# First stage of a long convolution: plain float32 fold, product on GpSimd, blocks made one ahead

## What is computed

```python
h_filt = (np.maximum(pos_emb @ w1, 0.0) @ w2) * window      # filter, 12480 x 128
u = x * v                                                   # 2 x 12480 x 128
y = irfft(rfft(u, 2 * S, axis=1) * rfft(h_filt, 2 * S, axis=0), axis=1)[:, :S]
x = (x * y).reshape(B * S, D)
h = x @ w_in
P = a[0] + a[1] * h + a[2] * h**2 + a[3] * h**3
Q = 1.0 + abs(b[0]) * abs(h) + abs(b[1]) * h**2
out = (P / (Q + 1e-6)) @ w_out
```

## Time and profile before

| | us |
|---|---|
| median of 3 runs | 2366.12 |
| lowest and highest run | 2360.96, 2369.22 |
| span of the profiled execution | 2364.7 |

### The profile page before, as it was taken

The page is one execution under the profiler, slowest core; times in us unless marked ns, Lnnn a source line. Parts: engine busy times, 40 slices in busy tenths (PEclk is TensorE's granted clock), DMA queues, the critical chain, the costliest instruction groups (busy, mean ns, idle before and its releaser), DMA issues.

```text
span 2364.7 us, 33272 instructions
## 1 busy us (share of the span) xinstructions
PE 2081.2 (88%) x8964; PEld 1464.9 (62%) x8964; DVE 2042.7 (86%) x2499; ACT 1993.8 (84%) x2670; POOL 1892.7 (80%) x1218
## 2 busy tenths in 40 slices
PE   7888578889877999999999999999999999999997
PEld 5666478889874555555555555555555555555554
DVE  3777566767666999999999999999999999999998
ACT  3677455555546999999999999999999999999998
POOL 3666367777755888888888888888888888888887
PEclk9999889999997999999999999999999999999999
DMA  6888655656552111111111111111111111111100
GB/s 163 246 257 263 206 128 146 154 139 162 137 127 60 29 29 28 28 31 28 31 48 28 28 28 28 28 28 28 31 28 32 48 28 28 28 28 28 28 11 11
DMA packets 65724, 175.02 MB, mean 74 GB/s; under 512 B 5046, under 2 KB 8414, under 8 KB 62686
## 3 DMA queue, kind: packets, MB, share of 16 engines
q1 hardware_dynamic: 65694, 174.67, 28.0%
HBM read 102.89 MB, written 71.76 MB: 74 GB/s over the span
## 4 chain that ended last, share of the span: by engine, by line
DVE 22%; ACT 20%; issue 11%; POOL 9%; PE 7%; ACTq 0%; DVEq 0%; DMA 0%; POOLq 0%
DVE g_s L735 9%; DVE lin L723 8%; ACT lin L634 6%; POOL den L609 6%; ACT mag L640 5%; ACT r_p L652 5%; DVE num L727 4%; PE m_p L790 3%; PE h_p L811 3%; POOL slope L601 3%; ACT den L645 3%; DVE xy_lo L714 1%; ACT xy_hi L625 0%; DVE oT L743 0%; ACT o_s L681 0%
## 5 line engine op out<-in xcount | busy, mean ns | idle before, releaser
L609 POOL TENSOR_TENSOR den<-slope,mag 128x832 f32<-128x832 f32 x480 | 944.6, 1968 | 43.4 <-POOL slope L601 6.9
L822 PE MATMUL acc_p<-g_s,w_out_s 128*128 128x416 f32 x1920 | 759.6, 518 | 18.3 <-DVE g_s L735 15.0
L601 POOL TENSOR_SCALAR slope<-mag,den_c 128x832 f32<-128x832 f32 x480 | 500.0, 1042 | 168.0 <-ACT mag L640 154.5
L723 DVE SCALAR_TENSOR_TENSOR lin<-lin,coef,h_p 128x832 f32<-128x832 f32 x480 | 516.4, 1076 | 33.9 <-ACT mag L640 33.9
L727 DVE SCALAR_TENSOR_TENSOR num<-lin,coef,h_p 128x832 f32<-128x832 f32 x480 | 518.8, 1081 | 17.0
L811 PE MATMUL h_p<-xy_hi,w_lo 128*128 128x416 f32 x960 | 406.5, 423 | 132.4 <-DVE num L727 110.2
L735 DVE SCALAR_TENSOR_TENSOR g_s<-num,coef,r_p 128x832 f32<-128x832 f32 x480 | 515.3, 1074 | 3.5 <-issue 1.8
L822 PEld LDWEIGHTS acc_p<-g_s,w_out_s 128*128 128x128 f32 x1920 | 346.9, 189 | 233.5 <-issue 210.8
L634 ACT ACTIVATE lin<-h_p,coef 128x832 f32<-128x832 f32 x480 | 458.0, 954 | 5.2 <-PE h_p L811 5.2
L645 ACT ACTIVATE den<-den 128x832 f32<-128x832 f32 x480 | 434.8, 906 | 27.4 <-POOL den L609 26.1
L811 PEld LDWEIGHTS h_p<-xy_hi,w_lo 128*128 128x128 f32 x960 | 180.7, 188 | 399.8 <-DVE num L727 384.2
(11 more groups left out here) (66 smaller groups left out, 2878.1 us busy)
## 6 DMA issues: line engine op xcount, KB each, us to landing
bent<-bent_s SPq DMA_DIRECT2D x60, 576.0 KB, 4.7
bin_s<-bent SPq DMA_DIRECT2D x24, 1440.0 KB, 12.6
x_s<-in_x SPq DMA_DIRECT2D x60, 416.0 KB
back<-back_s SPq DMA_DIRECT2D x24, 960.0 KB, 6.5
vin_s<-back SPq DMA_DIRECT2D x30, 768.0 KB, 5.8
v_s<-in_v SPq DMA_DIRECT2D x30, 416.0 KB
out<-o_s SPq DMA_DIRECT2D x60, 208.0 KB
pos_s<-in_pos_emb SPq DMA_DIRECT2D x30, 88.0 KB
```

What stands on the lines that cost most here:

```text
L601: nc.gpsimd.tensor_scalar(slope[:, q % DEEP], mag[:, q % DEEP], den_c[:, 1:2], den_c[:, 0:1], ALU.mult, ALU.add).then_inc(slope_done, 1)
L609: nc.gpsimd.tensor_tensor(den[:, q % DEEP], slope[:, q % DEEP], mag[:, q % DEEP], ALU.mult).then_inc(den_done, 1)
L723: nc.vector.scalar_tensor_tensor(out=lin[:, q % 2], in0=lin[:, q % 2], scalar=coef[:, 2:3], in1=h, op0=ALU.add, op1=ALU.mult).then_inc(qua ...
L822: mm = nc.tensor.matmul(acc_p[:, 0:TOK], w_out_s[:, ft], g_s[:, q % DEEP, t], start=(ft == 0), stop=(ft == FT - 1))
```

## The change

The fold takes plain float32 operands, one matmul for each half in place of three. The high and low copies of `fold` and `uh` and their four instructions per block are gone, with the two semaphores between them. The product runs on GpSimd. The preparation runs one block ahead (LEAD_MAKE 1) and the loads four (LEAD_LOAD 4). Fold 0 waits for the product and the filter of its block; product and filter wait for the folds of the block whose slot they overwrite. The thresholds of `split_done` in the later stages are two lower.

```diff
-            LEAD_LOAD, LEAD_MAKE, LEAD_SPLIT = 5, 2, 1
+            LEAD_LOAD, LEAD_MAKE = 4, 1
@@ gpsimd
-                def split_lo(i, s):
-                    for half in range(2):
-
-                        pool.wait_ge(uh_hi_done, (i * SLOTS + s) * 2 + half + 1)
-                        at = slice(half * (JB // 2), (half + 1) * (JB // 2))
-                        nc.gpsimd.tensor_tensor(uh_lo[:, s, at], uh[:, s, at], uh_hi[:, s, at].bitcast(F32),
-                                                ALU.subtract).then_inc(uh_lo_done, 1)
-
-                pipelined(pool, ITERS, SLOTS, [(0, split_lo)])
+                def product(i, s):
+                    blk = i * SLOTS + s
+                    pool.wait_ge(xv_in[s], 32 * (i + 1))
+                    if positive(blk - 1):
+                        pool.wait_ge(g_done, (blk - 1) * JB)
+                    nc.gpsimd.tensor_tensor(uh[:, s, :, 0:BD].rearrange("p j (b d) -> p b j d", b=BATCH),
+                                            x_s[:, s], v_s[:, s], ALU.mult).then_inc(prod_done, 1)
+
+                pool.wait_ge(pad_zero, SLOTS)
+                pipelined(pool, ITERS, SLOTS, [(LEAD_MAKE, product)])
@@ scalar
-                pipelined(act, ITERS, SLOTS, [(LEAD_MAKE, posT_copy), (0, cos_part(0)), (LEAD_SPLIT, split_hi(0)),
-                                              (LEAD_MAKE, relu), (0, cos_part(1)), (LEAD_SPLIT, split_hi(1)),
+                pipelined(act, ITERS, SLOTS, [(LEAD_MAKE, posT_copy), (0, cos_part(0)), (LEAD_MAKE, relu), (0, cos_part(1)),
                                               (0, cos_part(2)), (0, cos_part(3))])
@@ vector
                 def filt(i, s):
                     blk = i * SLOTS + s
                     dve.wait_ge(filt_ps, blk + 1)
+                    if positive(blk - 1):
+                        dve.wait_ge(g_done, (blk - 1) * JB)
...
-                pipelined(dve, ITERS, SLOTS, [(0, turn(0)), (LEAD_MAKE, product), (0, turn(1)), (LEAD_MAKE, filt),
-                                              (0, turn(2)), (0, turn(3))])
+                pipelined(dve, ITERS, SLOTS, [(0, turn(0)), (0, turn(1)), (LEAD_MAKE, filt), (0, turn(2)), (0, turn(3))])
@@ tensor
-                        if j % 2 == 0:
-                            pe.wait_ge(uh_lo_done, blk * 2 + j // 2 + 1)
+                        if j == 0:
+                            pe.wait_ge(prod_done, blk + 1)
+                            pe.wait_ge(filt_done, blk + 1)
                         pe.wait_ge(turned[j % 2], blk * (JB // 2) + j // 2)
                         for c in range(2):
-                            for n, (w, f) in enumerate(((fold_lo, uh_hi), (fold_hi, uh_hi), (fold_hi, uh_lo))):
-                                mm = nc.tensor.matmul(g_p[0:K1, j % 2, c, 0:COLS], w[:, c * K1:(c + 1) * K1], f[:, s, j, :],
-                                                      start=(n == 0), stop=(n == 2))
+                            mm = nc.tensor.matmul(g_p[0:K1, j % 2, c, 0:COLS], fold[:, c * K1:(c + 1) * K1], uh[:, s, j, :],
+                                                  start=True, stop=True)
                         mm.then_inc(g_done, 1)
```

More of the change, by code:

```diff
@@ L131, in hyena_mlp @@
             fold = sb("fold", [ROWS, 2 * K1])
-            fold_hi, fold_lo = sb("fold_hi", [ROWS, 2 * K1], F32R), sb("fold_lo", [ROWS, 2 * K1], F32R)
             turn_k = sb("turn_k", [K1, J, 3])
@@ L142, in hyena_mlp @@
             uh = sb("uh", [ROWS, SLOTS, JB, COLS])
-            uh_hi, uh_lo = sb("uh_hi", [ROWS, SLOTS, JB, COLS], F32R), sb("uh_lo", [ROWS, SLOTS, JB, COLS], F32R)
             part_s = sb("part_s", [K1, 2, 2, COLS])
@@ L152, in hyena_mlp @@
             xv_in, pos_in, bent_out = sems("xv_in"), sems("pos_in"), sems("bent_out", SLOTS * 2)
-            uh_hi_done, uh_lo_done = sem("uh_hi_done"), sem("uh_lo_done")
             pad_zero, prod_done, filt_done = sem("pad_zero"), sem("prod_done"), sem("filt_done")
@@ L227, in relu @@
                     nc.scalar.activation(hid[:], hid_p[:, 0:JB * FILTER_ROWS], ACT.Relu).then_inc(hid_sb, 1)
[L229 to L237, removed]
                 def cos_part(j):
@@ L248, in _ @@
                 act.wait_ge(consts_in, CONSTS)
-                nc.scalar.activation(fold_hi[:], fold[:], ACT.Copy).then_inc(split_done, 1)
-                pipelined(act, ITERS, SLOTS, [(LEAD_MAKE, posT_copy), (0, cos_part(0)), (LEAD_SPLIT, split_hi(0)),
-                                              (LEAD_MAKE, relu), (0, cos_part(1)), (LEAD_SPLIT, split_hi(1)),
+                pipelined(act, ITERS, SLOTS, [(LEAD_MAKE, posT_copy), (0, cos_part(0)), (LEAD_MAKE, relu), (0, cos_part(1)),
                                               (0, cos_part(2)), (0, cos_part(3))])
@@ L255, in _ @@
             def _(dve):
[L256 to L262, removed]
                 def filt(i, s):
@@ L288, in _ @@
                 dve.wait_ge(pad_zero, SLOTS)
-                dve.wait_ge(split_done, 1)
-                nc.vector.tensor_tensor(fold_lo[:], fold[:], fold_hi[:].bitcast(F32), ALU.subtract).then_inc(split_done, 1)
-                pipelined(dve, ITERS, SLOTS, [(0, turn(0)), (LEAD_MAKE, product), (0, turn(1)), (LEAD_MAKE, filt),
-                                              (0, turn(2)), (0, turn(3))])
+                pipelined(dve, ITERS, SLOTS, [(0, turn(0)), (0, turn(1)), (LEAD_MAKE, filt), (0, turn(2)), (0, turn(3))])
             @block.tensor
@@ L335, in _ @@
                 pe.wait_ge(consts_in, CONSTS)
-                pe.wait_ge(split_done, 2)
                 pipelined(pe, ITERS, SLOTS, [(LEAD_MAKE, transposes), (0, fold_j(0)), (LEAD_MAKE, hidden), (0, fold_j(1)),
@@ L476, in turn @@
                                                    ).then_inc(vturned[q % 2], 1)
-                dve.wait_ge(split_done, 4)
+                dve.wait_ge(split_done, 2)
                 nc.vector.tensor_tensor(spread_lo[:], spread_s[:], spread_hi[:].bitcast(F32), ALU.subtract).then_inc(split_done, 1)
@@ L512, in inverse @@
                     mm.then_inc(v_done, 1)
-                pe.wait_ge(split_done, 5)
+                pe.wait_ge(split_done, 3)
                 pipelined(pe, ITERS, PER, [(LEAD_FORWARD, forward), (LEAD_INVERSE, inverse)])
@@ L861, in step @@
                             turn_out(c, freed)
-                pe.wait_ge(split_done, 6)
+                pe.wait_ge(split_done, 4)
                 rows(0, 0, 0, 0, lambda: None)
```

## The result

Over 15 runs each, the median of the kernel before is 2363.49 us (2358.57 to 2370.29) and that of the changed one 2371.53 us (2368.71 to 2373.88): ratio 1.0031, with a 95% interval of 1.0021 to 1.0042. The change makes the kernel **8.0 us slower**. The forecast was no change, 2366.1 us, with a chance of 0.22 for slower. The measured time lies inside the range only because that reached up to 2379, for more blocks at TensorE's low clock in the changed kernel; it had one such block, as forecast.

A forecast was written before the change was run, and what follows sets the result against it. The prediction took a chain across engines to bound later first-stage blocks, TensorE alone the early ones. Terms -4.9, -5.0, +8.0, +1.5 and +0.4 us gave 0.0 on the profiled 2364.7; with 1.4 for the runs' median, 2366.1 us, range 2359.7 to 2379.

The forecast's parts named there:

- -5.0 on the first three blocks: Start of the first stage: 36.95 us before, 32.0 after, with one block at the low clock in place of three.
- the table load put at 0: Start of the first stage: removing ScalarE's split of the fold table was priced at 0, the load not being mentioned.
- the period: Time from one block's fold 0 to the next in the first stage: 8.54 us, bounds 8.50 to 8.68.
- The chain: First stage: fold 0, hidden matmul, fold 1, filter rows, fold 2, cos part and turn set a block, 0.33 us longer than before.
- The product on GpSimd: First stage: the product takes 2.45 us, at most 4.56, under a cover of 9.6, so it costs 0.
- One block ahead: Start of the first stage: preparing one block instead of two lets fold 0 start at 17.45, 4.9 us earlier.
- The split of the fold table lay under the wait for v: 0: Start of the first stage: removing this split neither gains nor costs time, as it was hidden behind a load.
- The low clock: Early blocks of the first stage: one slow block of 14.9 us after the change, where slow ones took 12.31 before.
- Before it was three: First stage of the kernel before: three blocks ran at TensorE's low clock, read from the first short fold matmul at 59.30.
- Rival A: Early blocks: more run at the low clock; two give +6.4 us (2372.5), three +12.7 (2378.8); chance 0.24.
- Rival B: Start of the first stage: the clock rises early, so no slow block, -6.4 us (2359.7); chance 0.07.
- Rival D: First stage: gaps between TensorE's jobs change, -9 to +9 us (2357 to 2375); chance 0.09.

The follow-up runs named there:

- after_dve: The changed kernel with the product x times v back on VectorE, between turn 0 and turn 1; median 2371.85 us, ratio to before 1.0042.
- after_twice: The changed kernel with the product made twice on GpSimd, first into an unread tile; median 2371.76 us, ratio to before 1.0039.
- after_table: The changed kernel plus an unused ScalarE copy of the fold table right behind the wait for the tables; median 2369.76 us, ratio to before 1.0035.
- after_late: The changed kernel with TensorE's filter rows behind fold 2 and VectorE's filter product behind turn 2; median 2370.14 us, ratio to before 1.0037.
- after_r: The changed kernel with three float32r matmuls per half, no split, low parts left out (other output); median 2351.64 us, ratio to before 0.9946.
- before_warm: The kernel before plus nine float32 matmuls on a constant tile at the start of TensorE's list; median 2361.94 us, ratio to before 1.0001.
- after_warm: The changed kernel plus nine float32 matmuls on a constant tile at the start of TensorE's list; median 2370.46 us, ratio to before 1.0042.

## Why the prediction was wrong

The step that failed is the term "-5.0 on the first three blocks". It took three blocks at the low clock, read from one execution, for what the kernel before has. Six executions had one to three, and the last turn ended at 276.7 in the mean, not at 280.0: 3.4 of the 5.0 are not there. Two smaller terms failed beside it, the table load put at 0 and the period; all are below.

- **The chain: right; the period: nearly, with some luck.** 8.54 forecast, 8.60 measured. Every start within the block came within 0.1. Three sizes were off, and the third takes back more than half of the other two. Fold 0 and fold 1 each hold TensorE 0.04 longer than forecast. A fold takes 1.53 from start to end, not 1.45. And fold 0 starts 0.06 behind the turn, not 0.15 or more, which takes 0.09 back. The 1.45 came from the matmuls of the earlier trace rows, which follow others without a gap; a pair of the same 416 columns that starts after a wait takes 0.10 longer than their 1.56 (the line from 1498.69 behind this list). Together 0.06 a block, 1.7 us in 28 blocks. That fold 0 waits for the turn holds although names GpSimd's subtraction in front of it (0.81 <-POOL uh_lo). The profile names it in every second block, but the distance from the end of the turn to fold 0 is 0.15 in both kinds, and the subtraction that ends there (98.59 to 100.41) is that of the block's second half, while fold 0 needs only the first.
- **The product on GpSimd: right** (2.35 for 2.45; cost 0, by after_dve and after_twice). The Trainium skill's advice against it (GPSIMD Engine Reference, section 4.1) did not matter here, as the rows had said: nothing on the chain waits for it.
- **One block ahead: right in kind, too large.** "The split of the fold table lay under the wait for v: 0" failed. That activation was ScalarE's first and carried the table load, 1.28 us, with it under the first transfers; without it the load stands behind the first transposes. By after_table that makes fold 0 start 1.5 us later, and 1.3 of these are the load.
- **The low clock: the count for the new kernel was right, the count for before was not typical.** "Before it was three" was true of one execution. The sum took 5.0 us of gain from it; against the mean of the six executions (276.7 in place of 280.0) it is 3.4 less. This is the largest part of the miss. That one block of the new kernel would be slow came true, but the reason given for it, the longer work of TensorE without a gap, was tested by no run.
- Together: 0.0 + 1.7 + 1.5 + 3.4 = 6.6, and 0.8 between the means of the second stage, which may be chance. That leaves under 1 of the 8.0, within the interval of the ratio (5.0 to 9.9 us). The changed kernel stands here with one profile, whose fold 0 was the latest of the four executions that start alike (19.12; 18.61, 18.75 and 18.22 in after_dve, after_twice and after_late), so each of these terms may be off by some tenths. The base of 2366.1 was itself 2.6 above the median of 15 runs.
- **Rival A** (more slow blocks, slower) gave 2372.5 for two of them, near the 2371.53 measured, but by luck: the changed kernel had one, and the count that varies is that of the kernel before. Rival B is refuted by every profile of the unfilled kernels: the first fold ran at the low level in all of them. The Trainium skill (TensorE: Matmul & The Clock Gate, Part 1) has sustained activity release the clock; the executions of before agree only in that it rises in the end, after 12, 25 or 37 us of busy folds. Rival D was right in kind for one gap, that of fold 0 behind its turn (0.15 to 0.06); the gaps between TensorE's own jobs stayed near 0.1, and its 9 us did not come.

The timeline of PE in the kernel before, for the first point:

```profile
1498.69 1.66 PE L822 MATMUL acc_p<-g_s,w_out_s 128*128 128x416 f32 x4 [0.27 <-DVE g_s L735]
```

## What to carry to other kernels

A forecast that takes a gain or a loss from a clock level must ask how often the kernel before has that level; one profile doesn't tell, and the runs' spread (12 us here) is a hint that it varies. When an instruction is removed, ask what came with it: here the first activation carried the table load. And before a change shortens a lead, look at which reorderings the longer lead allows: here moving one step in the old kernel gained 17 us, in the new one 1 or nothing.

## What the runs showed of the hardware

The column of the granted clock read 1.00 throughout the first stage, while the folds of the slow blocks ran at half speed for 12 to 37 us: the pitch of the matmuls is the sign to go by. In the six profiles of the unfilled or partly filled float32 kernels the clock was low in block 0 alone (in after_late in a part of it); the six executions of the float32r one had one to three slow blocks, and both after_r (two) and before_warm (one) fall in the same range. In after_warm a clock that had been high was low again after waits of 1.98 and 0.55 us in TensorE's work; with these waits filled it was high from the first fold on in all three kernels so made, each seen in one profile.
